# Merges of pairs of units by one product of 64 columns in a chunked delta rule, with the first step's units merged and scattered first

## The reference, cut to what matters

```python
def _attn_ref(q, k, v, beta):              # 4 x 8 heads, 768 positions, 48 wide
    k_n = k / (np.linalg.norm(k, axis=-1, keepdims=True) + 1e-06)
    state = np.zeros((B, H, D, D))
    for t in range(S):
        kt, vt, bt = k_n[:, :, t], v[:, :, t], beta[:, :, t, None]
        y[:, :, t] = einsum('bhd,bhde->bhe', q[:, :, t], state)
        v_old = einsum('bhde,bhd->bhe', state, kt)
        state = state + bt[..., None] * einsum('bhd,bhe->bhde', kt, vt - v_old)
# x = y as 3072 tokens of 384; then
# 8 experts: relu(x @ w1[e]) @ w2[e], weighed by P[:, e] (8 Sinkhorn rounds on exp(x @ w_gate))
# second layer: h = x @ w_in (2048 wide); (h * cos(h)) @ w_out
```

## Time and profile before

| | us |
|---|---|
| median of 3 runs (lowest to highest) | 2255.63 (2255.16 to 2255.84) |
| the profiled execution | 2254.29 |
| its span, first to last instruction | 2252.6 |
| PE busy | 2217.2 (98%) |
| DVE busy | 1024.7 (45%) |
| ACT busy | 721.9 (32%) |
| POOL busy | 507.9 (23%) |

### The profile page before, as it was taken

How to read it: one execution, slowest core, us unless ns; L and a number is a source line. 1 busy time by engine, 2 the same in 40 slices (tenths; PEclk the granted TensorE clock), 3 DMA queues, 4 the chain that set the end, 5 groups by cost and what they waited for, 6 DMA issues and landing times.

```text
span 2252.6 us, 40269 instructions
## 1 busy us (share of the span) xinstructions
PE 2217.2 (98%) x15520; PEld 1843.5 (82%) x15520; DVE 1024.7 (45%) x1744; ACT 721.9 (32%) x1153; POOL 507.9 (23%) x404
## 2 busy tenths in 40 slices
PE   5999999999999999999999999999999999999999
PEld 4888887888888888888888888888888888888887
DVE  8887734532323232322323232323223247777777
ACT  4555544111111111111111111111111226666665
POOL 1000001025423233232323232332323231000000
PEclk7899999999999999999999999999999999999999
DMA  4443343111110111111111111011111110000001
GB/s 122 99 96 94 93 109 106 43 40 46 30 45 28 33 28 33 28 33 41 31 30 29 32 28 47 28 33 28 31 30 28 47 24 14 15 14 15 0 15 70
DMA packets 81961, 97.68 MB, mean 43 GB/s; under 512 B 5696, under 2 KB 67456, under 8 KB 81856
## 3 DMA queue, kind: packets, MB, share of 16 engines
q1 hardware_dynamic: 81856, 96.18, 16.0%
HBM read 82.69 MB, written 8.75 MB: 41 GB/s over the span
## 4 chain that ended last, share of the span: by engine, by line
PE 95%; DVE 3%; ACT 1%; issue 1%; DVEq 0%
PE h L637 7%; PE h L638 7%; PE h L639 7%; PE p_h L637 7%; PE p_h L638 7%; PE p_h L639 7%; PE am_y L675 4%; PE am_y L676 4%; PE am_y L677 4%; PE chain_y L675 2%; PE chain_y L676 2%; PE chain_y L677 2%; PE o_y L675 2%; PE state_y L675 2%; PE o_y L676 2%; PE y_y L677 2%
## 5 line engine op out<-in xcount | busy, mean ns | idle before, releaser
L1166 POOL TENSOR_TENSOR acc<-acc,py 128x512 f32 (+1 forms) x252 | 324.3, 1318 | 746.6 <-DVE py L1467 746.6
L1031 ACT ACTIVATE hhi<-h 128x512 fp32r<-128x512 f32 x182 | 109.0, 599 | 769.5 <-PE h L639 769.5
L1430 DVE SCALAR_TENSOR_TENSOR hlo<-h,hhi 128x512 fp32r<-128x512 f32 x182 | 125.9, 692 | 477.6 <-ACT hhi L1031 477.6
L1430 DVE SCALAR_TENSOR_TENSOR hlo<-p_h,hhi 128x512 fp32r<-128x512 f32 x182 | 125.9, 692 | 404.5 <-ACT hhi L1031 404.5
L1128 POOL TENSOR_TENSOR wlo<-stage,whi (+1 forms) x114 | 147.1, 1292 | 644.7 <-ACT whi L909 619.0
L637 PE MATMUL p_h<-xhi,whi 128*128 (+1 forms) x690 | 268.8, 390 | 0.6 <-DVE scr L1527 0.6
L637 PE MATMUL h<-xhi,whi 128*128 (+1 forms) x690 | 268.7, 389 | 0.0
L638 PE MATMUL p_h<-xlo,whi 128*128 (+1 forms) x690 | 268.5, 389 | 0.0
L638 PE MATMUL h<-xlo,whi 128*128 (+1 forms) x690 | 268.4, 389 | 0.0
L639 PE MATMUL h<-xhi,wlo 128*128 (+1 forms) x690 | 268.4, 389 | 0.0
L639 PE MATMUL p_h<-xhi,wlo 128*128 (+1 forms) x690 | 268.4, 389 | 0.0
(11 more groups left out here) (254 smaller groups left out, 3990.8 us busy)
## 6 DMA issues: line engine op xcount, KB each, us to landing
stage<-wcat SPq DMA_DIRECT2D x38, 768.0 KB, 4.4
pb<-p_scratch SPq DMA_DIRECT2D x84, 256.0 KB, 4.7
kq<-kqt SPq DMA_DIRECT2D x48, 192.0 KB, 3.6
v<-vrow SPq DMA_DIRECT2D x24, 192.0 KB, 3.9
kb<-krow SPq DMA_DIRECT2D x24, 192.0 KB, 4.4
acc<-yT SPq DMA_DIRECT2D x72, 64.0 KB, 2.7
kT<-kta SPq DMA_DIRECT2D x20, 192.0 KB, 4.4
acc<-y_scratch SPq DMA_DIRECT2D x5, 768.0 KB, 4.6
```

The source lines that it names most:

```text
L1031: act.activation(hhi[:, j, :], hps[j % 2][:, 0:TILE], ACT.Relu).then_inc(s["hhi_done"], 1)
L1166: pool.tensor_tensor(y, y, py[:, d, :], ALU.add).then_inc(s["added"], 1)
L1430: dve.scalar_tensor_tensor(out=hlo[:, j, :], in0=hps[j % 2][:, 0:TILE], scalar=0.0, in1=hhi[:, j, :].bitcast(F32), op0=ALU.max, op1=ALU.su ...
```

## The change

- A merge takes two units in one product: the stationary operand is 64 columns (two units' blocks side by side) and the moving one 64 columns. Of the 64x64 result the two 32x32 blocks on the diagonal are used, the other two are thrown away. A merge of 16 units is 16 products in place of 32.
- A_ is laid out as two halves, so that two units' off-diagonal blocks are adjacent.
- The used blocks of the even and the odd units lie in different partitions. `merged_units` on ACT takes them out by four instructions of 32 partitions by 8 units of 32 (for b = 0, 1 and even, odd), for both stages, and the copy moves them to other partitions.
- DVE writes z_t first, with a semaphore of its own, and z_x behind it; stage 0 waits for z_t alone.
- The first group: units 0 to 7 (all that step (0, 0) reads) are merged and scattered ahead of step (0, 0). The other units' second half of the merge stands in step (0, 0) behind its w product, as does merge m = 2; m = 3 moves behind the step's output. Their copies and scatters on ACT move with them.
- Five warm-up products in place of eight; 12 filler products ahead of the first merges and 4 behind them in place of 16 ahead.

```diff
+        def merge_pairs(g, stg, bank, first, last):
+            for n in range(first, last, 2):
+                col = n % 16 * L
+                for b in range(2):
+                    lo, hi = b * CT, b * CT + L
+                    if stg == 0:
+                        mm = pe.matmul(rows(bank, b)[:, col:col + 2 * L], A_[lo:lo + L, g % 2, 1, n:n + 2, :].rearrange("p n i -> p (n i)"),
+                                       z_t[lo:lo + L, :, n:n + 2].rearrange("p j n -> p n j"), start=True, stop=True)
+                    else:
+                        mm = pe.matmul(rows(bank, b)[:, col:col + 2 * L], Y1[hi:hi + L, n:n + 2, :].rearrange("p n i -> p (n i)"),
+                                       z_x[hi:hi + L, :, n:n + 2].rearrange("p i n -> p n i"), start=True, stop=True)
+            return mm
...
+        def first_merges():
+            pe.wait_ge(a["zt_done"], 1)
+            pe.wait_ge(a["a_evac"], 8)
+            merge_pairs(0, 0, am_ps[0], 0, 8).then_inc(a["m_first"], 1)
+            merge_pairs(0, 0, am_ps[1], 8, 16).then_inc(a["m_first"], 1)
+            pe.wait_ge(a["z_done"], 1)
+            pe.wait_ge(a["m_firsted"], 1)
+            merge_pairs(0, 1, h_ps, 0, 8).then_inc(a["m_first"], 1)
+
+        def second_merge():
+            pe.wait_ge(a["m_firsted"], 3)
+            merge_pairs(0, 1, h_ps, 8, 16).then_inc(a["m_done"], 2)
...
+            if g == 0 and c == 0:
+                pe.wait_ge(a["m_firsted"], 2)
+                pe.wait_ge(a["sc_first"], 4)
...
+            if g == 0 and c == 0:
+                second_merge()
+                merge(0, 2)
...
+            if g == 0 and c == 0:
+                merge(0, 3)
...
-        for _ in range(8):
+        for _ in range(5):
...
-        unread(16)
-        for m in range(3):
-            merge(0, m)
+        unread(12)
+        first_merges()
+        unread(4)
...
+        def merged_units(g, stg, bank, first, last):
+            for b in range(2):
+                lo, hi = b * CT, b * CT + L
+                for odd in range(2):
+                    at = lo + odd * L
+                    came = bank[at:at + L, :].rearrange("p (n a i) -> p n a i", a=2, i=L)[:, first % 16 // 2:(last - 1) % 16 // 2 + 1, odd, :]
+                    units = slice(first + odd, last, 2)
+                    if stg == 0:
+                        ins = act.activation(Y1[hi:hi + L, units, :], came, ACT.Copy)
+                    else:
+                        ins = act.activation(X[lo:lo + L, g % 2, units, L:2 * L], came, ACT.Copy, scale=-1.0)
+            return ins
...
-            dve.transpose(z_x[:, :, :], t_leaf[:, :, :])
-            dve.transpose(z_t[:, :, :], t_leaf[:, :, :].rearrange("p i j -> p j i")).then_inc(a["z_done"], 1)
+            dve.transpose(z_t[:, :, :], t_leaf[:, :, :].rearrange("p i j -> p j i")).then_inc(a["zt_done"], 1)
+            dve.transpose(z_x[:, :, :], t_leaf[:, :, :]).then_inc(a["z_done"], 1)
```

More of the change, by code:

```diff
@@ L128, in build @@
     r = [w1_at]
-    A_ = inside(r, "A_", [P, 2, U, CT])
+    A_ = inside(r, "A_", [P, 2, 2, U, L])
     kT = inside(r, "kT", [P, U, CT])
@@ L433, in merge @@
             if m == 0:
+                pe.wait_ge(a["zt_done"], g + 1)
+            if m == 1:
                 pe.wait_ge(a["z_done"], g + 1)
@@ L441, in merge @@
                 pe.wait_ge(a["m_evac"], 4 * (g - 1) + 2 * k + 2)
[L442 to L452, removed]
+            merge_pairs(g, stg, am_ps[k], k * 16, (k + 1) * 16).then_inc(a["m_done"], 1)
+        def first_merges():
[9 more added lines that the diff above has]
+            merge_pairs(0, 1, h_ps, 8, 16).then_inc(a["m_done"], 2)
         def early_up(t, j):
@@ L558, in step @@
                 pe.wait_ge(a["r_done"], carried(g, c))
-            if c % 2 == 0:
+            if g == 0 and c == 0:
+                pe.wait_ge(a["m_firsted"], 2)
+                pe.wait_ge(a["sc_first"], 4)
+            elif g == 0 and c == 1:
+                pe.wait_ge(a["m_evac"], 2)
+                pe.wait_ge(a["sc_done"], 4)
+            elif c % 2 == 0:
                 pe.wait_ge(a["m_evac"], 4 * g + 2 + c)
@@ L570, in step @@
             beside_update(g, c)
-            if c == 0:
+            if g == 0 and c == 0:
+                second_merge()
+                merge(0, 2)
+            elif c == 0:
                 merge(g, 3)
@@ L795, in products @@
             act.wait_ge(a["a_done"], 4 * g + r + 1)
-            act.activation(A_[:, g % 2, r * RU:(r + 1) * RU, :], key_bank(g, r)[:, :].rearrange("p (n i) -> p n i", i=CT),
+            act.activation(A_[:, g % 2, :, r * RU:(r + 1) * RU, :].rearrange("p a n i -> p n a i"),
+                           key_bank(g, r)[:, :].rearrange("p (n a i) -> p n a i", a=2, i=L),
                            ACT.Copy).then_inc(a["a_evac"], 1)
@@ L813, in extract @@
             for q in range(4):
-                f = L * (q % 2)
-                act.activation(diag[L * q:L * q + L, :, :], A_[L * q:L * q + L, g % 2, :, f:f + L],
+                act.activation(diag[L * q:L * q + L, :, :], A_[L * q:L * q + L, g % 2, q % 2, :, :],
                                ACT.Copy).then_inc(a["ext_done"], 1)
@@ L825, in updates, with scatter_units @@
                            ACT.Copy).then_inc(a["w_evac"], 1)
+        def scatter_units(g, q, first, last):
+            f = L * (q % 2)
+            return act.activation(X[L * q:L * q + L, g % 2, first:last, f:f + L].rearrange("p n i -> p i n"),
+                                  z_x[L * q:L * q + L, :, first:last], ACT.Copy)
         def scatter(g, part, lo=0, hi=4):
@@ L829, in scatter @@
                 act.wait_ge(a["z_done"], g + 1)
-                if g == 0 and part == 0:
-                    act.wait_ge(a["x_zeroed"], 1)
                 if g >= 2:
                     act.wait_ge(a["w_done"], (g - 1) * STEPS)
-            n = slice(part * 16, part * 16 + 16)
             for q in range(lo, hi):
-                f = L * (q % 2)
-                act.activation(X[L * q:L * q + L, g % 2, n, f:f + L].rearrange("p n i -> p i n"), z_x[L * q:L * q + L, :, n],
-                               ACT.Copy).then_inc(a["sc_done"], 1)
+                scatter_units(g, q, part * 16, part * 16 + 16).then_inc(a["sc_done"], 1)
+        def merged_units(g, stg, bank, first, last):
[10 more added lines that the diff above has]
+            return ins
         def merged(g, m):
             k, stg = divmod(m, 2)
-            n = slice(k * 16, (k + 1) * 16)
             act.wait_ge(a["m_done"], 4 * g + m + 1)
[L844 to L851, removed]
+            merged_units(g, stg, am_ps[k], k * 16, (k + 1) * 16).then_inc(a["m_evac"], 1)
         def state(g, c):
@@ L943, in _ @@
             split_hi(0, chunk, 0, 1, wraw)
-        scatter(0, 0, 0, 1)
-        merged(0, 0)
+        act.wait_ge(a["m_first"], 1)
+        merged_units(0, 0, am_ps[0], 0, 8).then_inc(a["m_firsted"], 1)
+        act.wait_ge(a["z_done"], 1)
+        act.wait_ge(a["x_zeroed"], 1)
+        for q in range(2):
+            scatter_units(0, q, 0, 8).then_inc(a["sc_first"], 1)
+        act.wait_ge(a["m_first"], 3)
+        merged_units(0, 1, h_ps, 0, 8).then_inc(a["m_firsted"], 1)
         root(1)
-        scatter(0, 0, 1, 4)
-        merged(0, 1)
-        merged(0, 2)
+        for q in range(2, 4):
+            scatter_units(0, q, 0, 8).then_inc(a["sc_first"], 1)
+        merged_units(0, 0, am_ps[1], 8, 16).then_inc(a["m_firsted"], 1)
         for g in range(NG):
@@ L967, in _ @@
                         early_gate(g - 2)
-                    merged(g, 3)
+                    if g == 0:
+                        act.wait_ge(a["m_done"], 2)
+                        merged_units(0, 1, h_ps, 8, 16).then_inc(a["m_evac"], 2)
+                        for q in range(4):
+                            scatter_units(0, q, 8, 16).then_inc(a["sc_done"], 1)
+                        merged(0, 2)
+                    else:
+                        merged(g, 3)
                 if c == 1 and g >= 2:
@@ L980, in _ @@
                 if g == 0 and c == 0:
+                    merged(0, 3)
                     scatter(0, 1)
```

2 lines of the change are left out of this document (1 added, 1 removed).

## The result

The changed kernel takes 2264.56 us in the median (2263.77 to 2266.95), the kernel before 2255.74 (2253.42 to 2257.71) on the same chip, six runs each: 1.0039 times the time, interval 1.0027 to 1.0052. It is 8.8 us slower where 14.7 faster was forecast, and far outside the range of 2233 to 2250. The profiled execution took 2266.95 us (span 2265.2), 12.7 more than that of before: it is the slowest of its six, and that of before lies 1.4 under its median, so the profiles show some 4 us more of loss than the medians do.

What follows compares the result with a forecast made beforehand. PE's order was taken to set the time from step (1, 3) on. Merges 17.9 minus ACT waits 3.2 plus 0 for the start made 14.7 us less than 2254.3, 2239.6, as a median 2241; range 2233 to 2250.

Steps and rivals of the forecast that it cites:

- I take 0.98: it saves 0.94 a merge: Twenty merges of groups 1 to 5 on PE: each 0.98 us in place of 1.92 at full clock, 17.9 in all.
- The products gain nothing: Rival, chance 0.05: 64-column products cost twice 32-column ones, PE saves nothing, m = 0 copies cost 0.3 in three groups; 2256 to 2257.
- So the w product starts 4.0 us earlier: Step (0, 0): with half the merge and scatters ahead, ACT's list ends at 49.3 us, so its w product starts 4.0 earlier.
- I take nothing for the whole start: range from 3 us gained to 3 lost: Start and first step: work is only moved, R of (0, 1) at 66 to 68 us; 0, with 3 either way by clock.
- The copies on ACT: Merge copies become four of 0.38 us, 12.5 more on ACT; PE waits 1.25 in two groups and 0.7 in one, 3.2.
- it mostly has slack: ACT, 32% busy over the span, was taken to have slack except where someone waits for what is behind the merge copies.
- the three places searched: Copies ahead of the hidden value (3.2 us lost), m = 2 copy ahead of step 0's W (nothing), stage 1 copies (hidden).
- wrong if PE waited for S anywhere: Sign that the forecast is wrong: PE waits for S; the stage 1 copies ahead of the S copy were counted as hidden.
- The clock gets worse: Rival: new PE waits bring low-clock stretches; one or two give 2245 to 2248 us (0.14), six more 2262 (much worse, 0.07).
- the clock gets better: Rival, chance 0.20: new merges have more columns in less time, falls at 97.7 and 131.8 go; 6 us less, 2235.

Runs made afterwards that it cites:

- a1_forms: The changed kernel with the merge's product in another form in each group, numbers wrong from group 2 on; one execution, 2261.91 us.
- a2: The changed kernel with PE's wait for the gate's low part moved to the first gate products in group 2; 2261.46 us, 1.0034 of the kernel before.
- c2: c1 with PE's wait for the gate's low part moved to group 2; 2253.84 us, 0.9996 of the kernel before.
- c1: The changed kernel with merges reading adjacent pairs of moving elements, output and copies permuted to match; 2256.66 us, 1.0004 of the kernel before.
- a4: The changed kernel with the old 32x32 merge products and whole copies, its first step kept; 2255.41 us, 1.0006 of the kernel before.
- b1: The kernel before with z_x and z_t written unit by unit, so merges and scatters read adjacent elements; 2244.99 us, 0.9954 of the kernel before.

## Why the prediction was wrong

**"I take 0.98: it saves 0.94 a merge" (wrong, the largest term).** Measured: 1.90 us, so 0.02 saved. 19 x 0.02 + 0.07 makes 0.4 us of the 17.9. The rows that it was taken from, key and query products, differ from the merge in the number of rows and in something that the shapes in the profile do not show: the step between moving elements. a1_forms shows that the step is the cause. The rows could have raised the doubt: the old merge took 1.94 us at 1.2 GHz and 1.92 at 2.4, while the query products took 1.87 against 1.05. A time that is the same at both clocks has another limit than the clock, and the forecast read from these rows only that a merge at low clock gains little.

**"The products gain nothing" (right on PE's time, wrong in cause and total).** This rival had the sum of the merges right and put the time at 2256 to 2257. That a product of 64 columns costs twice one of 32 came out as it says, but for the step and not for the width: with 64 adjacent columns the 16 products take 1.08 us. A rule of the Trainium skill stood behind it ("TensorE: Matmul & The Clock Gate", section "LDWEIGHTS (loading the stationary operand)"), by which the forecast estimated 53 ns for a load of 64 columns. It does not bound the merge here: with adjacent elements the same 32 records, each with a load of 64 columns, follow at 1.07 us / 32 = 33 ns. What carried the time from there to 2264 was the first step, the clock and some waits.

**"So the w product starts 4.0 us earlier" (wrong: a missed wait).** The count went along ACT's list, which was nearly right: in a2 the product starts at 50.12 with its operand, 3.2 earlier than before, and in c2 at 49.07. It left out that PE waits for wgr ahead of all steps, done at 52.78. Before, that wait lay hidden, since the product began at 53.28. It cost 2 to 3 us (a2 2.4, c2 against c1 2.8), and started the product only 0.4 earlier.

**"I take nothing for the whole start: range from 3 us gained to 3 lost" (wrong in size).** R of (0, 1) came at 72.00, against 66 to 68. From W of (0, 0) the count allowed some 15 to 17 us to it, and it took 17.1. The late start explains 3.6 of the 5; no row shows a single cause for the rest. Then step (0, 1) ran at the low level, which the lower end of the range was meant for, and the loss was 9.6 us at (0, 3), of which 4.7 came back by (1, 3). In a4 the first step's loss, 3.6 us at (0, 1), is paid back in full.

**"The copies on ACT": prices right, the slack wrong.** 374 ns was as forecast. In c2, where the merge is near the forecast's price, a single wait in (2, 3) was 1.10 us against 1.25. But "it mostly has slack" and the three places searched missed that ACT's work also passes through DVE: the hidden value released late makes the leaf chain late, and that makes the expert weights' low parts late. Waits of 9.7 us where 3.2 were counted; c2 shows this in full, since in the changed kernel merges never became short enough. The forecast also called itself wrong if PE waited for S anywhere: it did, twice, 0.8 us in all, in the changed kernel and in c2.

**"The clock gets worse": right in part.** Between (1, 3) and (5, 3) three falls of 3.4 us, some 1.6 each, make 4.8 of the 7.4 us lost there. PE's waits in that stretch, 1.3 for hlo, 0.8 for S and 0.7 more than before for wlo, make another 2.8, and with that the 7.4 are accounted for. The forecast asked for four stretches more to lose all gain; with the gain absent, three small ones and a longer first one sufficed. Which gap causes which fall stays open. The other clock rival, "the clock gets better", rested on more columns in less time; a new merge has as many as an old one, 2048, in nearly the same time, 1.90 us against 1.92.

## What to carry to other kernels

Before a product's price is taken from another product, compare the step of the moving operand in memory as well as the shapes, and check whether the old time changed with the clock: one that does not has another limit, which a new shape may keep. When a product is brought forward, list every semaphore that its engine waits for ahead of it, also those that belong to something else. A gain on the bound engine counts only up to where the other engines' own order arrives; follow that chain through two engines, not one.

## What the hardware showed

- A moving operand of fp32 with 32 elements (128 bytes) from column to column took 0.93 ns a column at 2.4 GHz and 0.95 at 1.2 (1.94 us for 2048), so the faster clock gave next to nothing. With adjacent pairs it did: 1.90 us at 1.2 GHz (c1) and 1.07 at 2.4 for a merge of 32 records, as good as 1.08 with 64 adjacent (a1_forms).
- ACT's copy of 32x512 from `stage` to X: 1106 ns with its writes 64 elements apart (before), 628 ns with reads and writes in runs of 32 adjacent elements (b1).
- DVE's transpose of 128x1024 took 2017 ns with z_x written in steps of 32 elements (b1), 1245 with no steps (before). That of z_t, which reads in steps in both, took 1978 ns before and 2044 with steps on its output too (b1).
